# An attention stage on one Trainium2 core: the accumulator leaves by ScalarE alone, the tail's transposes stand ahead of the values, and one score take is split in two

## What is computed

```python
q_pool = q.reshape(B, H, S // 2, 2, D).mean(axis=3)          # B, H, S, D = 4, 8, 1152, 64
scores = scale * np.matmul(q_pool, k.transpose(0, 1, 3, 2))  # 576 x 1152 for each head
scores = scores - np.max(scores, axis=-1, keepdims=True)
attn = np.exp(scores)
attn = attn / (np.sum(attn, axis=-1, keepdims=True) + 1e-09)
attn_out = np.matmul(attn, v)                                # 576 x 64 for each head
...
x = _moe_ref(x=attn_out, ...)      # gated MLP with a spatial gate
return _moe2_ref(x=x, ...)         # token mixing, then channel mixing
```

## Time and profile before

| | |
|---|---|
| timed runs, median (all) | 1016.01 us (1016.01, 1012.86, 1016.03) |
| the profiled execution's own time | 1012.23 us |
| its span | 1010.4 us |
| PE busy, of the span | 986.5 us |
| DVE, ACT, POOL busy | 583.0, 447.4, 382.2 us |
| attention (to about 434 us) | 16 pairs; a middle pair takes 25.9 to 26.0 us |

### The profile page before, as it was taken

How to read it: one execution, slowest core, us unless ns; L and a number is a source line. 1 busy time by engine, 2 the same in 40 slices (tenths; PEclk the granted TensorE clock), 3 DMA queues, 4 the chain that set the end, 5 groups by cost and what they waited for, 6 DMA issues and landing times.

```text
span 1010.4 us, 22952 instructions
## 1 busy us (share of the span) xinstructions
PE 986.5 (98%) x8898; PEld 812.6 (80%) x8898; DVE 583.0 (58%) x1157; ACT 447.4 (44%) x848; POOL 382.2 (38%) x297
## 2 busy tenths in 40 slices
PE   6999999999999999999999999999999999999998
PEld 5776777777777766679999999988888888888898
DVE  6788777777787777789494957654213113121121
ACT  4777777777777777755151514232111101111111
POOL 4876777777777778640000103386000000000000
PEclk8999999999999999999999999999999999999999
DMA  5644444444444432320000000142001001000010
GB/s 183 181 119 118 117 109 113 117 117 117 117 117 117 115 93 64 110 95 6 1 2 1 1 1 24 32 137 84 1 0 42 1 1 42 0 7 35 0 42 21
DMA packets 34475, 65.55 MB, mean 65 GB/s; under 512 B 6272, under 2 KB 15360, under 8 KB 34432
## 3 DMA queue, kind: packets, MB, share of 16 engines
q1 hardware_dynamic: 33984, 64.37, 22.4%
q10 hardware_dynamic: 448, 0.56, 0.2%
HBM read 42.93 MB, written 4.72 MB: 47 GB/s over the span
## 4 chain that ended last, share of the span: by engine, by line
PE 88%; issue 5%; DVE 3%; POOL 1%; DMA 1%; ACT 1%; SPq 0%; DVEq 0%; ACTq 0%; POOLq 0%
PE ps L824 18%; PE ps L826 18%; PE ps L825 18%; PE ps L780 12%; PE ps L763 10%; PE ps L708 6%; DVE prob L1317 2%; PE ps L746 1%; DVE pT L1332 1%; PE ps L747 1%; PE ps L748 1%; PE ps L877 1%; DMA k_over<-kl 1%; POOL prob L595 0%; DMA k_two<-in_k 0%
## 5 line engine op out<-in xcount | busy, mean ns | idle before, releaser
L1317 DVE TENSOR_SCALAR_CACHE_REDUCE prob<-ps 128x1152 f32<-128x1152 f32 x144 | 195.3, 1357 | 71.2 <-PE ps L763 51.3
L595 POOL TENSOR_SCALAR prob<-prob,rsum 128x1152 f32<-128x1152 f32 x144 | 177.9, 1236 | 112.3 <-DVE rsum L1326 111.9
L1104 ACT ACTIVATE prob<-prob,nmax 128x1152 f32<-128x1152 f32 x144 | 181.0, 1257 | 6.6
L780 PE MATMUL ps<-pT,v_sb 128*64 128x288 f32 x1152 | 170.6, 418 | 2.0
L1563 DVE SCALAR_TENSOR_TENSOR f_l<-ps,f_h 128x512 fp32r<-128x512 f32 (+1 forms) x60 | 38.3, 638 | 222.5 <-ACT f_h L1266 222.5
L1090 ACT ACTIVATE pT<-ps 128x512 f32<-128x512 f32 (+1 forms) x288 | 109.5, 432 | 98.6 <-PE ps L708 98.6
L1266 ACT ACTIVATE f_h<-ps 128x512 fp32r<-128x512 f32 (+1 forms) x60 | 33.3, 555 | 254.8 <-PE ps L826 254.8
L763 PE MATMUL ps<-k_over,q_over 64*128 64x288 f32 x744 | 131.1, 309 | 0.2 <-DMA k_over<-kl 0.2
L763 PEld LDWEIGHTS ps<-k_over,q_over 64*128 64x128 f32 x744 | 102.2, 185 | 20.1 <-DVE prob L1317 19.3
L708 PEld LDWEIGHTS ps<-ident,prob 64*128 64x128 f32 x2592 | 99.6, 139 | 22.6 <-issue 22.6
L708 PE MATMUL ps<-ident,prob 64*128 64x64 f32 x2592 | 107.5, 224 | 8.3 <-DVE prob L1317 3.6
(11 more groups left out here) (157 smaller groups left out, 2137.3 us busy)
## 6 DMA issues: line engine op xcount, KB each, us to landing
q_raw<-in_q SPq DMA_DIRECT2D x16, 640.0 KB, 5.1
k_raw<-in_k SPq DMA_DIRECT2D x16, 576.0 KB, 4.0
v_sb<-in_v SPq DMA_DIRECT2D x32, 288.0 KB, 2.9
k_over<-kh SPq DMA_DIRECT2D x31, 144.0 KB, 2.5
k_over<-kl SPq DMA_DIRECT2D x31, 144.0 KB, 2.6
out_x<-xT SPq DMA_DIRECT2D x4, 1024.0 KB, 4.2
q_over<-qh SPq DMA_DIRECT2D x31, 128.0 KB, 2.2
q_over<-ql SPq DMA_DIRECT2D x31, 128.0 KB, 2.3
```

Source lines behind the costliest of these rows:

```text
L595: g.tensor_scalar(sl, sl, rsum[:, s:s + 1], 0.0, ALU.mult, ALU.add).then_inc(norm_done, 1)
L780: ins = te.matmul(ps[PH * c:PH * c + PH, ACC_BANK, 0:n], v_sb[:, a, j, :], pT[:, a, j, c * n:c * n + n], start=(j == 0), stop=(j == KB - 1))
L1104: sc.activation(sl, sl, ACT.Exp, scale=-1.0, bias=nmax[:, s:s + 1], accum_out=esum[:, s:s + 1]).then_inc(exp_done, 1)
L1317: ve.tensor_scalar(prob[:, PROB_BUF[s], :].rearrange("p (c n) -> p c n", c=SCORE_BANKS), ps[:, b0:b0 + SCORE_BANKS, 0:CK], -SCALE, BIG, AL ...
```

## The change

It has three parts.

1. `acc_copy` is done by ScalarE alone, in two copies one behind the other, in steps 3 and 8 and once more at the end of the attention stage. The two semaphores acc_by_act and acc_by_dve become one, acc_moved, and VectorE's copies go.
2. In the last step T comes ahead of V, as in the other steps. ScalarE's copy of the last key block and VectorE's copy of the tail now wait for the V that is behind T; ScalarE's first copy (head 0's part) waits for nothing but the transposes.
3. The take of step 3, the one that the tail's scores wait for, is done in two instructions of 128 x 576 elements, two banks each, and a third of 128 x 1 that forms the minimum of the two. The tail's scores wait for the first half ahead of bank 0, and for the second half ahead of bank 2.

```diff
@@ -422,12 +423,11 @@
             return SCORE_BANKS * (s % 2) if s < LAG else 0
-        def pT_free(eng, i, s):
-            if s == 0 and not (isinstance(i, int) and i == 0):
-                eng.wait_ge(acc_ready, at(i, 4, -2))
-            if s in (TAIL_STEP, TAIL_STEP + 1) and not (isinstance(i, int) and i == 0):
-                eng.wait_ge(acc_ready, at(i, 4, 0))
+        def pT_free(eng, i, a):
+            if not (isinstance(i, int) and i == 0):
+                eng.wait_ge(acc_ready, at(i, 4, 2 * a - 2))
         def load_two(eng, rows):
...
@@ -737,11 +735,13 @@
                 if first and s < LAG:
                     if s >= 2:
                         pe.wait_ge(s_taken, s - 1)
-                else:
+                elif s != TAIL_STEP:
                     pe.wait_ge(s_taken, at(i, NS, s))
                 if s == TAIL_STEP:
                     tail = slice(4 * P, QC)
                     for c in range(SCORE_BANKS):
+                        if c % 2 == 0:
+                            pe.wait_ge(half_taken, at(i, 2, c // 2 + 1))
                         cols = slice(c * CK, (c + 1) * CK)
                         te.matmul(ps[:, c, 0:CK], qh2[:, par, tail], kh2[:, par, cols], start=True, stop=False)
                         te.matmul(ps[:, c, 0:CK], qh2[:, par, tail], kl2[:, par, cols], start=False, stop=False)
...
@@ -768,8 +768,7 @@
                 if js[0] == 0:
                     if not (isinstance(i, int) and i + a == 0):
-                        pe.wait_ge(acc_by_act, at(i, 2, a))
-                        pe.wait_ge(acc_by_dve, at(i, 2, a))
+                        pe.wait_ge(acc_moved, at(i, 4, 2 * a))
                     last = TAIL_STEP if a == 0 else NS - 1
                     pe.wait_ge(pT_by_dve, at(i, NS, last + 1))
                     pe.wait_ge(pT_by_act, at(i, 2 * NS, 2 * last + 2))
...
@@ -784,16 +783,13 @@
             def step(i, par, s, first=False, tail=False):
-                pv_first = s == NS - 1
-                if pv_first and not first:
-                    values(i - 1, *PV_STEPS[s])
                 if s >= LAG and not tail:
                     if first and s == LAG:
                         pe.wait_ge(s_taken, LAG)
                     transpose_p(i, s - LAG)
                 elif s < LAG and not first:
                     transpose_p(i - 1, s - LAG + NS)
-                if not pv_first and not first:
+                if not first:
                     values(i - 1, *PV_STEPS[s])
                 if not tail:
                     scores(i, par, s, first)
...
@@ -1107,14 +1102,19 @@
             def evac_p(i, s):
                 act.wait_ge(p_ready, at(i, 2 * NS, 2 * s + 2))
-                pT_free(act, i, s)
+                if s in (0, TAIL_STEP + 1):
+                    pT_free(act, i, head_of(s))
                 copy(pT_of(s, 0), trans(0)).then_inc(pT_by_act, 1)
+                if s == TAIL_STEP:
+                    pT_free(act, i, 1)
                 copy(last_of(s), ps[:, LAST_BANK, 0:P].rearrange("p (h q) -> p h q", h=2)).then_inc(pT_by_act, 1)
             def acc_copy(i, a):
                 act.wait_ge(acc_ready, at(i, 4, 2 * a + 2))
-                copy(xT[PH * a:PH * a + PH, i, 0:HALF], ps[0:PH, ACC_BANK, 0:HALF]).then_inc(acc_by_act, 1)
+                for c in range(2):
+                    copy(xT[PH * a:PH * a + PH, i, c * HALF:(c + 1) * HALF],
+                         ps[PH * c:PH * c + PH, ACC_BANK, 0:HALF]).then_inc(acc_moved, 1)
             def step(i, s, first=False, tail=False):
...
@@ -1314,6 +1314,16 @@
                     dve.wait_ge(p_ready, at(i + before[0], 2 * NS, 2 * before[1] + 2))
                 dve.wait_ge(s_ready, at(i, 2 * NS, 2 * s + 2))
                 b0 = first_bank(s) if isinstance(i, int) and i == 0 else 0
+                if s == TAIL_STEP - 1:
+                    for m in range(2):
+                        cols = slice(m * 2 * CK, (m + 1) * 2 * CK)
+                        ve.tensor_scalar(prob[:, PROB_BUF[s], cols].rearrange("p (c n) -> p c n", c=2),
+                                         ps[:, b0 + 2 * m:b0 + 2 * m + 2, 0:CK], -SCALE, BIG, ALU.mult, ALU.min,
+                                         accum_out=nmax_half[:, m:m + 1]).then_inc(half_taken, 1)
+                    dve.wait_ge(half_taken, at(i, 2, 2))
+                    ve.tensor_tensor(nmax[:, s:s + 1], nmax_half[:, 0:1], nmax_half[:, 1:2], ALU.min).then_inc(s_taken, 1)
+                    return
                 ve.tensor_scalar(prob[:, PROB_BUF[s], :].rearrange("p (c n) -> p c n", c=SCORE_BANKS),
                                  ps[:, b0:b0 + SCORE_BANKS, 0:CK], -SCALE, BIG, ALU.mult, ALU.min,
                                  accum_out=nmax[:, s:s + 1]).then_inc(s_taken, 1)
...
@@ -1328,13 +1338,9 @@
             def evac_p(i, s):
                 dve.wait_ge(p_ready, at(i, 2 * NS, 2 * s + 2))
-                pT_free(dve, i, s)
+                if s in (0, TAIL_STEP, TAIL_STEP + 1):
+                    pT_free(dve, i, head_of(s))
                 ve.tensor_copy(pT_of(s, 1), trans(1)).then_inc(pT_by_dve, 1)
-            def acc_copy(i, a):
-                dve.wait_ge(acc_ready, at(i, 4, 2 * a + 2))
-                ve.tensor_copy(xT[PH * a:PH * a + PH, i, HALF:SQ], ps[PH:P, ACC_BANK, 0:HALF]).then_inc(acc_by_dve, 1)
             def step(i, s, first=False, tail=False):
...
@@ -1346,8 +1352,6 @@
                     recip(i, s - 2)
                 elif s < 2 and not first:
                     recip(i - 1, s - 2 + NS)
-                if not first and s in (TAIL_STEP - 1, NS - 1):
-                    acc_copy(i - 1, 0 if s == TAIL_STEP - 1 else 1)
                 if not tail:
                     take(i, s)
                     if first and 2 <= s < LAG:
```

More of the change, by code:

```diff
@@ L142, in build @@
         nmax = sb(ctx1, "nmax", [P, NS])
+        nmax_half = sb(ctx1, "nmax_half", [P, 2])
         esum = sb(ctx1, "esum", [P, NS])
@@ L236, in build @@
         s_taken = sem("s_taken")
+        half_taken = sem("half_taken")
         exp_done = sem("exp_done")
@@ L244, in build @@
         acc_ready = sem("acc_ready")
-        acc_by_act = sem("acc_by_act")
-        acc_by_dve = sem("acc_by_dve")
+        acc_moved = sem("acc_moved")
         sgT_hi = sem("sgT_hi")
@@ L521, in _ @@
                 load_w(u)
-            sp.wait_ge(acc_by_act, 2 * NP)
-            sp.wait_ge(acc_by_dve, 2 * NP)
+            sp.wait_ge(acc_moved, 4 * NP)
             sp.dma_start(b_row[:, :], b_sg.partition_broadcast(P)).then_inc(small_in, 16)
@@ L658, in _ @@
             norm_rstd(0, 1)
-            pool.wait_ge(acc_by_act, 2 * NP)
-            pool.wait_ge(acc_by_dve, 2 * NP)
+            pool.wait_ge(acc_moved, 4 * NP)
             for u in range(U_WO, U_T1):
@@ L841, in v_tile @@
                     if b == 0:
-                        pe.wait_ge(acc_by_act, 2 * NP)
-                        pe.wait_ge(acc_by_dve, 2 * NP)
+                        pe.wait_ge(acc_moved, 4 * NP)
                     pe.wait_ge(res_done, 4 * b + RES_N - 1)
@@ L1513, in _ @@
             gelu(0, 1)
-            acc_copy(NP - 1, 1)
+            dve.wait_ge(acc_moved, 4 * NP)
             sg_lo(4)
```

## The result

The changed kernel takes 1024.21 us (median of 6 runs, 1022.59 to 1027.21), the kernel before 1014.42 in the same comparison (6 runs, 1012.80 to 1016.03): ratio 1.0102, 95% interval 1.0087 to 1.0116, about 10 us slower. Forecast were 1007.5 us, a range of 1002.5 to 1013.5 and a chance of 0.77 for faster. The profiled execution took 1024.88 us, with a span of 1022.8.

The account below looks back on a forecast made before the run. TensorE's waits in attention, chiefly the tail's scores for VectorE's take, were to be cut: 6.0 + 0.45 + 0.45 - 0.3 = 6.6 us. That gave 1005.6 (profiled) or 1009.4 (median); 1007.5 was chosen, range 1002.5 to 1013.5.

Parts of the forecast that it names:

- What it costs elsewhere: Side effects on VectorE, ScalarE and GpSimd in attention: the minimum makes later VectorE work some 0.25 us later, all covered.
- The cover that I had counted for T of step 5: Spare time between VectorE's copy and the transposes of step 5: 0.6 us.
- The tail's wait: In step 4 the tail's scores wait for VectorE's take: 0.40 us gained in each of 15 pairs, 6.0 us.
- Part 1's share of it: Gain ahead of the tail's scores from dropping VectorE's accumulator copy: 0.11 us a pair (0.03 to 0.18).
- A half take at 0.75: VectorE's take of 576 elements in step 3 was estimated at 0.75 us, against 1.36 for the whole.
- One wait less in front of V: Before the values products of steps 4 and 0, one of five waits goes: 0.45 us in all (0 to 0.9).
- The last step and step 0: Reordered last step brings the next step 0's transposes earlier: 0.03 us a pair, 0.45 us in all (0 to 1.8).
- the whole gap at step 0 closes: Rival: step 0's transposes waited only for ScalarE, so 0.27 us a pair goes, 3.6 us more gain; chance 0.08.
- The start: In pair 0 the take of step 3 has no cover; the second instruction and minimum lose 0.3 us.
- Given back downstream: Rival: step 4's 0.40 us returns as a wait of step 5's transposes or a late take; chance 0.07.
- The clock rival: Rival: longer TensorE idling at the start prolongs the low clock, up to 6 us more, gain gone; chance 0.04.
- two levels: Three timed runs of the kernel before, 1012.86, 1016.01 and 1016.03 us, read as two levels 3.2 us apart.

Follow-up runs that it names:

- e1: Changed kernel with the minimum of the two halves as a one-input reduction instead of a two-input operation: 1006.29 us, ratio 0.9926 to the kernel before.
- e2: Changed kernel, two-input minimum kept, with GpSimd's low part of k one step later: 1005.41 us, ratio 0.9911 to the kernel before.
- e3: Kernel before plus one unread two-input 128x1 minimum on VectorE behind the take of step 3: 1026.74 us, ratio 1.0131.
- p3_halves_one_input: Kernel before with only the take in halves (part 3), its minimum a one-input reduction: 1007.30 us, ratio 0.9949.
- p1_acc_by_act: Kernel before with only part 1, both accumulator copies by ScalarE: 1012.87 us, ratio 0.9987.
- p12_parts_1_and_2: Kernel before with parts 1 and 2, without the halves of the take: 1007.90 us, ratio 0.9941.
- p2_tail_first: Kernel before with only part 2, the tail's transposes ahead of the values in the last step: 1011.08 us, ratio 0.9977.
- e5: Changed kernel, two-input minimum kept, with GpSimd's low part of k issued as two 128x576 instructions: 1008.68 us, ratio 0.9956 to the kernel before.
- e6: Changed kernel with both the one-input reduction and GpSimd's low part of k one step later: 1005.79 us, ratio 0.9931 to the kernel before.

## Why the prediction was wrong

**The step that failed** is in "What it costs elsewhere": "The minimum of the halves (143 ns by its like ..., some 0.2 with its wait)", and behind it "None of this costs anything". The like was the addition of line 1324, which has one input in SBUF; the minimum has two, and starts 0.55 us after a GpSimd instruction of 2.67 us. It takes 2.12 us. Experiments e1, e2 and e3 show that it takes both: with one input, or with GpSimd idle, it is 0.16 us, and in the kernel before the same instruction by itself costs 12.7 us. The cover that I had counted for T of step 5, 0.6 us on VectorE's copy, was right: e1_min_one_input has the copy's end at 202.21 and T at 202.93, 0.72 later, of which 0.10 is the way from copy to T. So 0.62 is covered, and 2.12 - 0.16 - 0.62 = 1.34 isn't; measured are 1.30 a pair, 18 us in 14 pairs. No other loss is needed: with it gone the kernel is 7.5 us faster than before.

**The trace of before could have told.** Its pair loop has no VectorE instruction with two SBUF inputs, which is why the pairs show no such case, but the start has (timeline, VectorE and GpSimd of the kernel before):

```profile
11.87 2.65 POOL L588 TENSOR_TENSOR kl<-k_raw,kh 128x1152 fp32r<-128x1152 f32 x1 [1.55 <-ACT kh L1090]
13.31 1.89 DVE L1302 TENSOR_TENSOR q_sum<-q_raw 128x640 f32<-128x640 f32 x1
14.50 1.79 POOL L595 TENSOR_SCALAR prob<-prob,rsum 128x1152 f32<-128x1152 f32 x1
16.91 1.31 POOL L595 TENSOR_SCALAR prob<-prob,rsum 128x1152 f32<-128x1152 f32 x1 [0.62 <-DVE rsum L1326]
17.16 1.73 DVE L1307 TENSOR_TENSOR ql<-q_sum,qh 128x640 fp32r<-128x640 f32 x1
```

An addition of 128x640 takes 1.89 us, while line 1296, two SBUF inputs at 128x576, takes 0.755 in the same trace. GpSimd's instruction ends at 14.52, the addition 0.68 later at 15.20; in the second case 18.22 and 18.89, 0.67. And the lock seems to work both ways: GpSimd's multiplication that is due at 14.50 takes 1.79 us, where 144 of its kind average 1.236. In e2_low_k_later's trace GpSimd's low part of k happens to end at 13.86, ahead of the same addition, which then takes 0.80 (line 1296's own view in the kernel before, then line 1302 in the timeline of e2_low_k_later):

```profile
L1296 DVE TENSOR_TENSOR kl_two<-k_two,kh_two x2: 751/755/759, 7.0 to 7.7; 128x576 fp32r<-128x576 f32 x2
14.21 0.80 DVE L1302 TENSOR_TENSOR q_sum<-q_raw 128x640 f32<-128x640 f32 x1
```

**The other terms.**
- The tail's wait: 0.40 a pair forecast, 0.32 measured, in the whole change and in p3_halves_one_input (V to the tail's scores 0.64 in both, 0.96 before, where 0.56 was forecast; what holds the last 0.08 stays open). Part 1's share of it is as forecast: T4 to S4 is 0.11 shorter in p1_acc_by_act.
- A half take at 0.75: right.
- One wait less in front of V (0.45 in all): not seen, V of step 4 stands 0.80 behind T as before. Why p3_halves_one_input has 0.72 there in every second pair, which is the rest of its 0.40 from T4 to S4, stays open.
- The last step and step 0: 0.03 a pair forecast, 0.29 measured in e1_min_one_input and p12_parts_1_and_2 (8.97 to 8.68). The mechanism was half right: VectorE's copy did wait for V (1.33 from V's start at 215.25 in p2_tail_first) and T for the copy, but T follows this copy after 0.10, not 0.22. In the kernel before it was ScalarE's pair of copies that held T, as the profile's releaser had it: they end at 216.91 (line below), and T follows at 217.05, 0.14 later, as p1_acc_by_act's does (218.36, 218.50). That is the premise of the rival "the whole gap at step 0 closes", and of the gap of 0.27 part 2 closed 0.17. And what the accumulator's copy does to V of step 0 was set down as nothing.

```profile
216.14 0.77 ACT L1090 ACTIVATE pT<-ps 128x512 f32<-128x512 f32 x2 [1.73 <-PE ps L708]
```

- The start: 0.3 lost forecast, 0.27 measured. From the start of pair 0's take of step 3 to its T there are 1.77 us (14.87 to 16.64), before 1.50 (15.12 to 16.62). T stands at nearly the same time only because VectorE came to this take 0.25 earlier in this execution.

The sum, 6.6 us, is near the 7.5 to 7.8 us of e1_min_one_input, but that is partly luck. By the pair 0.46 was forecast and 0.65 measured: the tail 0.08 too high, the wait in front of V 0.03 too high, the last step 0.26 too low. And 14 pairs at 0.65 would be 9.1 us; in the profiled execution the last two pairs win only 0.4 each, and the tail's scores of pair 1 come 0.8 later (49.23 instead of 48.45), of which the 0.27 of the start are a part.

The rivals had a late minimum in none of them, and the chance of 0.07 for slower stood for other mechanisms. "Given back downstream" named the place, T of step 5 waiting for a copy, and asked for one estimate to be out by 0.8 us; the minimum was out by 1.9 (2.12 instead of 0.2). The clock rival isn't what made the loss: timed runs of the changed kernel at a mean granted clock of 0.997 took 1022.9 and 1023.5 us, some 10 us more than the kernel before at 0.996 to 0.998 (1012.0 to 1013.5). In its profiled execution the granted clock did fall a second time near the start (0.50 from 26 to 28 us, 1.00 there before), and from the tail's scores of pair 0 to those of pair 1 it took 31.3 us instead of 29.5; e1_min_one_input, whose start differs in the minimum alone, took 29.8. That is a part of why the profiled executions differ by 12.4 us of span where the medians differ by 9.8.

## What to carry to other kernels

An instruction that the kernel doesn't have yet is priced by a like instruction in engine, operand places and neighbours, not in size: count its SBUF inputs, and look what GpSimd runs when it starts. On VectorE beside a busy GpSimd, write two-operand work of one column as a reduction over adjacent columns or with a per-partition scalar (larger forms weren't tried); in the profile the fault shows as a long duration with no idle time ahead of it, and its end equals that of a GpSimd row. A delay costs what is left of it behind its cover: 2 us more than counted with 0.6 of cover cost 1.3 a pair, an added instruction of 0.88 us without cover cost 0.8.

## What else the runs showed

The runs of one kernel differ by some 3 us, and go with the mean granted clock of the execution: of 17 runs of the kernel before, those at a clock of 0.996 to 0.998 took 1012.0 to 1013.5 us, those at 0.989 to 0.991 1014.4 to 1015.7 (the runs beside p2, p3, e5 and e6). In 12 of the 13 profiled executions all that is missing of the full clock is missing in the first 40 us:

```profile
0.00:40.00 40.00, 30.64 (x378) 27.46 (x380) 25.68 (x55) 20.92 (x37) 24.69 (x25) 0.91 0.64 196
```

is the kernel before (profiled at 1012.23 us), with a granted clock of 0.91 there, and e6_both's profiled execution has

```profile
0.00:40.00 40.00, 31.77 (x338) 29.80 (x340) 23.23 (x55) 19.50 (x33) 21.90 (x23) 0.74 0.57 173
```

The exception is e2_low_k_later's profiled execution (1010.38 us, where its other runs took 1003.6 to 1006.0). It has 0.79 in the first 40 us and a second low stretch in the last pair, behind 2.7 us in which TensorE waited for GpSimd's multiplication (GpSimd had waited 4.0 us for a DMA of the next stage's weights):

```profile
404.00:406.00 2.00, 1.35 (x20) 1.27 (x22) 0.09 (x1) 0.09 (x1) 2.00 (x3) 0.51 0.00 0
```

So the "two levels" of the forecast are one kernel whose granted clock is at its upper level sooner or later, mostly at the start, and the medians of the timed runs, not the profiled executions, are what is to be compared. What decides it wasn't tried.
